# Split weights kept in DRAM for a second batch, block sums in place in PSUM, GpSimd for all low parts of weights

## What is computed

```python
# attention: B=2, H=8, S=768, D=64; window 16, blocks of 32
k_sum = k.reshape(B, H, nb, 32, D).max(axis=3); v_sum = v.reshape(B, H, nb, 32, D).mean(axis=3)
a = softmax(concat(mask(q @ k.T / sqrt(D)), q @ k_sum.T / sqrt(D) + log(32)))
x = a @ concat(v, v_sum)                     # -> [2, 768, 512]
# first block: w_tok1 768x256, w_tok2 256x768, w_ch1 512x1536, w_ch2 1536x512
u = x + (relu(x.T @ w_tok1) @ w_tok2).T
x = u + relu(u @ w_ch1) @ w_ch2
# second block: w_ch1 512x2048, w_ch2 2048x512
xn = (x - mean(x)) / sqrt(var(x) + 1e-6) * g
out = x + relu(xn @ w_ch1) @ w_ch2
```

## Time and profile before

| | before |
|---|---|
| median of three runs | 644.25 us |
| the profiled execution | 643.52 us |
| its span | 641.7 us |
| mean granted clock of TensorE | 0.965 |
| TensorE busy | 592.1 us (92%), 2976 matmuls |
| VectorE busy | 356.0 us (55%) |
| ScalarE busy | 244.5 us (38%) |
| GpSimd busy | 291.2 us (45%) |
| moved by DMA | 50.34 MB, mean 78 GB/s |

### The profile page before, as it was taken

The page is one execution under the profiler, slowest core; times in us unless marked ns, Lnnn a source line. Parts: engine busy times, 40 slices in busy tenths (PEclk is TensorE's granted clock), DMA queues, the critical chain, the costliest instruction groups (busy, mean ns, idle before and its releaser), DMA issues.

```text
span 641.7 us, 8274 instructions
## 1 busy us (share of the span) xinstructions
PE 592.1 (92%) x2976; PEld 512.1 (80%) x2976; DVE 356.0 (55%) x675; ACT 244.5 (38%) x450; POOL 291.2 (45%) x267
## 2 busy tenths in 40 slices
PE   5989999858999989799989979999899989999998
PEld 2777888647888878688878868888799868989896
DVE  6577665335544548784463878444635664444435
ACT  3577664422333234244423423333324323333321
POOL 5365653274444457534454843444561843333300
PEclk9899999887999989899998979999989989999999
DMA  8977722000311011112110111111101111111302
GB/s 232 243 221 203 213 61 78 0 1 5 121 54 56 30 65 66 65 51 82 65 42 25 66 65 66 67 65 66 65 2 66 66 66 65 66 66 65 132 1 99
DMA packets 24896, 50.34 MB, mean 78 GB/s; under 512 B 7596, under 2 KB 7832, under 8 KB 24856
## 3 DMA queue, kind: packets, MB, share of 16 engines
q1 hardware_dynamic: 24304, 49.37, 23.6%
q10 hardware_dynamic: 552, 0.44, 0.3%
HBM read 46.07 MB, written 3.15 MB: 77 GB/s over the span
## 4 chain that ended last, share of the span: by engine, by line
PE 70%; DVE 13%; POOL 6%; issue 4%; ACT 4%; DMA 2%; SPq 1%; DVEq 0%; POOLq 0%; ACTq 0%
PE bank L500 67%; DVE hidden L989 5%; POOL in_t L453 3%; DVE down_w L914 2%; PE bank L593 2%; DMA tok_stage<-w_tok 1%; ACT hidden L828 1%; ACT in_t L806 1%; DMA k_sb<-k_w 1%; DVE neg_scores L932 1%; DVE c_raw L1086 1%; DVE c_raw L1072 1%; ACT probs L755 1%; DVE k_sb L920 1%; PE bank L535 0%
## 5 line engine op out<-in xcount | busy, mean ns | idle before, releaser
L500 PE MATMUL bank<-down_w,hidden 128*128 128x512 f32 x1008 | 277.1, 404 | 5.3 <-issue 3.1
L500 PEld LDWEIGHTS bank<-down_w,hidden 128*128 128x128 f32 x1008 | 190.0, 193 | 34.0 <-issue 6.6
L500 PE MATMUL bank<-in_t,up_even 128*128 128x384 f32 x588 | 121.9, 344 | 10.7 <-ACT p L834 6.0
L500 PE MATMUL bank<-in_t,up_odd 128*128 128x384 f32 x588 | 123.2, 346 | 7.5 <-DVE c_raw L1086 7.5
L500 PEld LDWEIGHTS bank<-in_t,up_even 128*128 128x128 f32 x588 | 107.4, 192 | 20.5 <-ACT p L834 6.4
L500 PEld LDWEIGHTS bank<-in_t,up_odd 128*128 128x128 f32 x588 | 108.4, 193 | 17.8 <-issue 8.7
L828 ACT ACTIVATE hidden<-c_raw 128x384 fp32r<-128x384 f32 x84 | 44.1, 525 | 176.9 <-DVE c_raw L1072 85.1
L989 DVE SCALAR_TENSOR_TENSOR hidden<-c_raw,hidden 128x384 fp32r<-128x384 f32 x84 | 75.9, 903 | 39.4 <-ACT hidden L828 39.4
L422 POOL TENSOR_TENSOR up_even<-sums_up,up_even 128x1024 fp32r<-128x1024 f32 x14 | 33.6, 2401 | 120.5 <-ACT up_even L818 120.4
L422 POOL TENSOR_TENSOR up_odd<-sums_up,up_odd 128x1024 fp32r<-128x1024 f32 x14 | 33.5, 2392 | 98.5 <-ACT up_odd L818 98.5
L1042 DVE TENSOR_TENSOR u<-bank,p 128x384 f32<-128x384 f32 x28 | 15.6, 557 | 88.3 <-PE bank L500 80.5
(11 more groups left out here) (89 smaller groups left out, 758.4 us busy)
## 6 DMA issues: line engine op xcount, KB each, us to landing
raw_up<-w_ch SPq DMA_DIRECT2D x28, 512.0 KB, 4.3
raw_down<-w_ch SPq DMA_DIRECT2D x28, 512.0 KB, 3.5
k_sb<-k_w SPq DMA_DIRECT2D x16, 273.0 KB, 4.7
v_own<-v_w SPq DMA_DIRECT2D x8, 390.0 KB, 3.1
q_sb<-q_t SPq DMA_DIRECT2D x8, 384.0 KB, 5.7
v_turned<-v_t SPq DMA_DIRECT2D x8, 384.0 KB, 4.3
out<-natural SPq DMA_DIRECT2D x12, 256.0 KB, 3.1
tok_stage<-w_tok SPq DMA_DIRECT2D x4, 384.0 KB, 5.3
```

Source lines behind the costliest of these rows:

```text
L500: return nc.tensor.matmul(dst, lhs, rhs, start=start, stop=stop, skip_group_check=True)
```

## The change

1. **Kept weights.** Only groups 0 and 2 load, sum, cast and split the first matrix's weights (14 of 28 pairs, `is_made`). SP then copies the finished `up_w` (7 blocks, high and low, 1.84 MB) of each to a DRAM tensor `up_kept` (`keep_up`). In groups 1 and 3 it is read back from there in one transfer (`load_again`), which waits until the pair two ahead has made its products. The second matrix's weights are loaded, cast and split for each pair as before.
2. **Block sums in place.** `add_c` writes the sums back into the product's bank, `c_raw` is gone, and ScalarE and VectorE read the hidden blocks from PSUM. P6 starts its bank anew, and P4 is added to `u2` on VectorE. TensorE's waits for `c_made` become waits for `hid_low`.
3. **Low parts.** `low_up` and `low_down` move from VectorE to GpSimd, and all seven input low parts of groups 1 to 3 are GpSimd's. ScalarE casts some earlier or later to suit.
4. **Batch 0's inputs** are turned tile by tile (`first_tile`, four transposes) in tiles 43 to 47 of attention and behind it; their four sums and seven low parts are VectorE's (`sum_first`, `low_first`), three of the low parts within pair 0. What was made for pair 1's weights in attention (casts, low parts) moves into pair 0.

The core of the diff (the definitions of the moved steps are the same but for the engine and counts):

```diff
+            def keep_up(q):
+                sp.dma_start(up_kept[nth_made(q)], up_w[q % 2].bitcast(F32).rearrange("p s a c -> p (s a c)")
+                             ).then_inc(kept[q % 2], 16)
+
+            def load_again(q):
+                g, j = group_of(q)
+                sp.wait_ge(up_done, 7 * (q - 1))
+                last = nth_made(q - 2) if j < 2 else nth_again(q)
+                sp.wait_ge(kept[q % 2], 16 * (last // 2 + 1))
+                sp.dma_start(up_w[q % 2].bitcast(F32).rearrange("p s a c -> p (s a c)"), up_kept[nth_again(q)]
+                             ).then_inc(ld_again[q % 2], 16)
...
+            def make_group(g):
+                for q in range(FIRST[g], FIRST[g] + PAIRS_OF[g]):
+                    sp.wait_ge(raw_low, nth_made(q) + 1)
+                    sp.wait_ge(sums_low, nth_made(q) + 1)
+                    if q + 2 < FIRST[g] + PAIRS_OF[g]:
+                        load_up(q + 2)
+                    elif g == 0:
+                        load_up(FIRST[2] + q + 2 - FIRST[1])
+                    keep_up(q)
+                    if q + 2 < FIRST[g] + PAIRS_OF[g]:
+                        load_down(q + 2)
+
+            def repeat_group(g):
+                for q in range(FIRST[g], FIRST[g] + PAIRS_OF[g]):
+                    load_down(q)
+                    load_again(q)
...
@@ pool
-            for q in range(1, NQ):
+            for q in range(NQ):
                 g, j = group_of(q)
-                if j == 0:
+                making = q + 1 < NQ and is_made(q + 1)
+                if g and j == 0:
                     for i in range(LATE_IN, 7):
                         low_input(g, i)
-                if q + 1 < NQ:
+                if making and q and q + 1 != FIRST[2]:
                     sum_weights(q + 1)
+                if making:
+                    low_up(q + 1)
+                low_down(q)
+                if making:
                     low_sums(q + 1)
+                if g == 1 and j == 2:
+                    sum_weights(FIRST[2])
...
@@ tensor
+                if n >= TURN0:
+                    first_tile(n - TURN0)
...
                     if i == 6:
-                        pe.wait_ge(c_made, 3 * q + 1)
+                        pe.wait_ge(hid_low, 4 * q + 2)
...
                     if b < 2:
-                        pe.wait_ge(c_made, 3 * q + 2 + b)
+                        pe.wait_ge(hid_low, 4 * q + 3 + b)
...
@@ vector
+            def add_c(q, k, i, u):
+                c = product_bank(q, i)[:, 0:HN]
+                dve.wait_ge(up_done, 7 * q + i + 1)
+                dve.wait_ge(u_made, 3 * q + 3)
+                nc.vector.tensor_tensor(c, c, u[:], ALU.add).then_inc(c_made, 1)
...
-                nc.vector.tensor_tensor(c_raw[:, 0], product_bank(q, 4)[:, 0:HN], u3[:], ALU.add).then_inc(c_made, 1)
-                low_hidden(q, 1, c_raw[:, 0])
+                nc.vector.tensor_tensor(u2[:], product_bank(q, 4)[:, 0:HN], u2[:], ALU.add).then_inc(u_made, 1)
+                add_c(q, 0, 4, u3)
+                low_hidden(q, 1, product_bank(q, 4)[:, 0:HN])
```

341 lines of the change are left out of this document (185 added, 156 removed).

## The result

The changed kernel takes **611.56 us**, the median of four runs (610.57 to 613.67), against 644.05 us for the kernel before (643.22 to 644.62): a ratio of 0.950, 95% interval 0.947 to 0.953. The profiled execution took 611.47 us with a span of 609.7; before it was 643.52 and 641.7. The forecast was 607, its range 600 to 622.

A forecast was written before the change was run, and what follows sets the result against it. TensorE, nearly gapless, was taken as the floor, with 37.5 us lost around three changes of group. From 643.5, terms -17, -37.5, +7.8, +3, +6.6 and +0.1 sum to -36.9; with 0.7 for the median, 607 us, range 600 to 622.

The forecast's parts named there:

- End of attention, -17: From attention's last tiles to pair 1's start: batch 0's inputs turned in attention save 17 us (bounds -13 and -19).
- Losses removed, -37.5: Pairs 1 to 26: 37.5 us lost around the three changes of group fall away with remainders on GpSimd, sums in bank.
- Bank held longer, +7.8: P6 waits for P4's block remainder: 0.15 us a pair, 0.5 with turned batches; 7.8 us in all (bounds 0 and 16).
- Opening pairs, +3: VectorE's other work delays sums: 0.5 us each in pairs 6, 7, 12, 20, 1.0 in 13; +3 (0 to 8).
- GpSimd at group 2, +6.6: Start of group 2: GpSimd late by 2.1 us at pair 12's P0, 3.0 at pair 13's P1; +6.6 (2 to 12).
- Keeping at no cost: Writing and rereading 1.84 MB of weights for 14 pairs stays hidden on the queue, 7.3 to 12.2 us each: cost 0.
- A PSUM source: Skill's table gives PSUM sources 62 cycles more than SBUF; by it the sum would be 1.7 us higher; not adopted.
- Banks binding harder: Rival: handovers cost 0.1 more or P6 and next products all wait, 16 us for 7.8; 615 to 622, chance 0.12.
- GpSimd's stalls: Rival: GpSimd's steps wait at each group change and after, about half of 37.5 stays; 622 to 636, chance 0.07.
- The queue: Rival: at 150 GB/s the DMA queue bounds made pairs at 19.2 us each; 640 us, chance 0.03.
- The clock: Rival: TensorE's clock falls to 1.2 GHz after each pair's short wait, 1.8 us a pair; 654 us, chance 0.04.
- signs of being wrong: Pair 1 after 148, made pairs over 18 us, ragged clock behind 150 us, or pairs 6, 7, 20 near 19 us.

The follow-up runs named there:

- The last two timelines: Pair 3 in two kernels: the changed one with weights' remainders back on VectorE, 626.81 us; the same plus all three added block sums in SBUF, 639.74 us.
- the first two experiments: Changed kernel with all three added block sums in one SBUF buffer, 606.56 us; changed kernel with only P4's sum in SBUF, 602.70 us.
- the third experiment: Changed kernel with pair 12's weight sums cast earlier and their remainder put ahead of down_w's in pair 11: 606.12 us.
- the fastest kernel: Changed kernel with P4's block sum in SBUF and pair 12's weight sums cast early, both together: 597.75 us.

## Why the prediction was right, and where its sizes were off

**End of attention, -17, was -14.1.** The mechanism is the one given: the `x_split` remainder took 0.56 us, the clock fall and the 6.00 us wait are gone, and the wait for `h_tok` is 1.07 us where 1.3 was allowed. Two things were left out. The transposes of four tiles stand ahead of `x_split` on TensorE, 0.60 us each in the rows and about 0.4 from their start to the next one; from the `h_tok` matmuls behind tile 42 to `x_split` TensorE needs 8.17 us where it was ready after 6.85 before. I had started from the 2.96 us wait as if only the remainder stood there. And pair 1 waits 0.96 us for the last `hidden` remainder of pair 0, which is the bank held longer, a term that I had applied from pair 2 on. The rest is spread: TensorE got to the last tiles 1.5 us later in this profile (those `h_tok` matmuls begin at 108.38, in the trace of before at 106.88). Pair 0 starts between 126.08 and 127.78 in the seven profiles of kernels that are alike up to there, with 126.48 in their middle, so about 1 us of this term is no more than that. With these, nine `x_split` matmuls began at 116.55 where 114.8 was predicted.

**Losses removed, -37.5, held as a whole.** No remainder of a hidden block takes over 0.56 us, and TensorE has no wait on a sum. The 37.5 itself is taken as a whole in the table; no row measures it apart from the three lines below it. "The copy in SBUF is slowed when GpSimd works" was the right row read too softly. The last two timelines show what it is: two steps with both operands in SBUF, one on VectorE and one on GpSimd, don't share, the one that starts second stands until the first is done. This is the rule in the Trainium skill, page "SBUF — State Buffer", section "Who interferes with whom": an exclusive lock between the two for such steps, and issue order decides who blocks. The rows agree within 0.2 us, in both orders, and so do all 25 meetings of these two steps in the two traces: the second step ends 2.24 to 2.26 us behind the first where it is GpSimd's, 1.08 or 1.09 where it is VectorE's. By it the collision is to be looked for at every pair of overlapping steps, and its price is the rest of the other's step, up to 2.4 us here.

The kernel before fits it too. GpSimd's step against the 2.15 us remainder of the earlier trace rows was a sum of inputs, not of weights:

```profile
223.07 2.67 POOL L441 TENSOR_TENSOR t_in<-raw_in 128x768 f32<-128x768 f32 x1
```

It started 0.93 us ahead of the remainder at 224.00, and the remainder ended 0.41 us behind it.

What the prediction did not take apart is that a part of the 37.5 was the clock. Pairs 1 to 26 as windows, before and in the changed kernel:

```profile
159.54:614.43 454.89, 432.13 (x2101) 381.89 (x2101) 256.32 (x360) 161.08 (x257) 209.48 (x153) 0.97 0.18 63
```

```profile
145.48:581.88 436.40, 429.00 (x2101) 371.02 (x2101) 172.10 (x329) 136.52 (x229) 210.60 (x132) 1.00 0.44 161
```

TensorE was idle for 22.8 us, and in six stretches with or behind waits of 2.0 to 3.1 us its granted clock was 0.50, for 27.3 us in all (from 226.2, 267.1, 335.4, 376.4, 465.1 and 519.7). Half of that, 13.7 us, is what they cost as an estimate, and 22.8 + 13.7 = 36.5 is nearly the 37.5. In the changed kernel there is no such stretch behind pair 1's start. So more than a third of this term is the clock, gone together with the waits that it fell with: each such stretch cost another 1.7 or 3.4 us on top of its wait.

How the 37.5 divide is another matter than I implied when I put both parts of the edit under one term. With all else as changed, both undone cost 28.2 us, the remainders of weights alone 15.2, and the sums in place alone are worth *minus* 5.0. With the remainders on VectorE the sums in place are worth 639.7 - 626.8 = 12.9. Sums in place are needed only where VectorE also has long steps with both operands in SBUF; once those are on GpSimd, nothing is queued behind VectorE's slow steps. And "pairs of groups 1 and 3 gain nothing of their own" from keeping was true of the pairs inside them, but their starts would have kept 10.5 us.

**Bank held longer, +7.8, was +11.1.** A pair is 0.31 us longer, not 0.15. P6's start did slip by what was worked out, 0.16 us: P5 to P6 is 1.90 us in pair 24 where it was 1.74, with 0.10 us between the two adds on VectorE for which I took the 0.03 of a handover, and 0.06 in place of 0.1 to reach TensorE. What the term lacked is that P6's first weight load then has nothing to hide behind: its second matmul starts 0.28 us after the first, in place of 0.175, so another 0.10. The remaining 0.06 is in the first two experiments too, where P6 does not wait, so it is not the bank's. With a turned batch it was 0.59 where 0.5 was taken. The bounds of 0 and 16 held it.

**Opening pairs, +3, were +3.1.** Pairs 6 and 7 had 0.28 and 0.46 of the 0.5 each, pair 20 (16.00 us) none. Pairs 12, 13 and 14 keep 0.3, 0.6 and 1.0 with GpSimd's work out of their way (the third experiment); the 1.0 is the delay of pair 13 that was put at 1.0, shown one pair later. The size is right, and its places only in part.

**GpSimd at group 2, +6.6, was +4.8.** The wait at P0 of pair 12 is 2.15 us where 2.1 was worked out, and the third experiment removed it by moving the sums' cast, as that working says. In pair 13 it was waits of 0.63 us at P0, 0.92 at the first unit of `down` (for GpSimd's `down_w`) and 0.80 at P1, 2.4 together and not one of 3.0. The 1.5 that the term holds beyond 2.1 and 3.0 is for a fall of the clock, which this profile does not have (granted 1.00 from 331 to 345 us). In the run that writes weights twice there was one behind the same wait, 0.50 from 334.4 to 337.8, and it cost nothing: pairs 12 and 13 take 35.5 us together in both. That TensorE has to wait for GpSimd either way would explain it; it was not tried.

**Keeping at no cost** held: 8.1 us for a write and 7.3 for a read, against the 7.3 to 12.2 given. The estimate of 6.2 us by the Trainium skill, "DMA: Bandwidth & Descriptors", was too low for this queue by 1.9 and 1.1 us; nothing hung on either.

**A PSUM source**, which costs 0.065 us more by the table of the Trainium skill, "VectorE: DVE Perf Modes", errata section, cost nothing more here: remainders take 557 ns from the bank and 0.56 us from `c_raw` undisturbed. The place of the result made no odds either: sums take 559 ns in place and 556 into SBUF.

**The rivals.** Banks binding harder would have been 16 us and were 11.1. GpSimd's stalls are one wait of 2.15 us on `in_t` and those of 0.92 and 0.80 us on remainders of weights. The queue had room for 1.84 MB more in a pair that makes weights. The clock did not fall behind the start of the pairs in the profiled execution, with waits of 0.4 to 0.6 us ahead of weight loads in every pair (the four executions have a mean of 0.986 to 0.994), so the rule on depth-cycling (the Trainium skill, "TensorE: Matmul & The Clock Gate") has no case in the changed kernel's pairs. Closest to one is the run with batch 0's tiles turned behind attention, where the clock fell among waits of 0.68 us.

**The signs.** `hidden<-bank` at 557 ns in all 112, and no wait on a reload, came as said, and so did P6's slip, 0.16 us (0.1 to 0.2 given). Pair 1 at 145.48 (142 to 144 given) and pairs of 16.0 and 17.0 us (15.8 to 15.9 and 16.9) missed on the late side. None of the signs of being wrong came. That 607 was met within 5 us owes something to luck as well: what GpSimd's term had too much, 1.8 us, covered a part of the 6.2 by which the two others were short.

**Still open** is how the 37.5 us of the kernel before divide between its own collisions, as the kernel with both edits undone is not that kernel: its made pairs lose time inside the groups, those of the kernel before mostly around the changes of group, where GpSimd sums inputs. Nor was it tried what is left in pairs 14 and 10 (17.74 and 17.50 us) of the fastest kernel.

## What to carry to other kernels

Where VectorE and GpSimd both work on operands in SBUF, lay their steps side by side in time and look at which starts first: the second one pays the rest of the first, and a shift of 0.2 us of one against the other moved 2 us from the engine that had time to the one that was waited for. Moving results to PSUM avoids it but holds the bank for the whole chain behind it, so do it only for the results whose bank is not wanted next. Look at the granted clock behind each long wait of TensorE too, for a wait can cost more than its length: here 22.8 us of idle time came with 27.3 us at half clock. And when a loss is cured by two edits at once, undo each alone before carrying both on: here one of them was worth 15 us with the other in place, and the other, once the first was made, cost 5 to 9.

## What the runs showed of the hardware that I had not expected

- VectorE's and GpSimd's two-operand steps in SBUF exclude each other nearly in whole: 1.22 us and 3.35 (alone 2.41) with VectorE 0.11 us ahead, 2.40 and 3.37 (alone 1.22) with GpSimd 0.12 us ahead.
- TensorE's granted clock was 0.50 for 3.4 or 6.8 us with or behind waits of 2.0 to 3.1 us (six times in pairs 1 to 26 of the kernel before, 27.3 us), behind a wait of 2.15 us in one trace and not in another, and not once behind waits of 0.4 to 0.6 us in pairs of 16 and 17 us.
- A VectorE add that depends on the VectorE step before starts 0.10 us behind its end, an independent one 0.08 us ahead of it.
- A weight load that starts late is not hidden: P6's second matmul starts 0.28 us after its first where its load waited for the bank, 0.175 where it did not.
- An add from PSUM into PSUM (559 ns) costs the same as one into SBUF (556), for 384 elements a partition.
- The queue carried 4.72 MB in a pair of 17.0 us, 277 GB/s, beside all other work, with no change to these pairs.
